# Scores of the first two head pairs: two matmuls a tile on keys where they land, in place of one on laid-out keys

## What is computed

```python
k_sum = k.reshape(B, H, nb, 32, D).max(axis=3)       # maxima of 24 blocks of 32 keys
v_sum = v.reshape(B, H, nb, 32, D).mean(axis=3)
scores_l = scale * q @ k.T        # kept only where |i - j| < 16
scores_s = scale * q @ k_sum.T + log(32)
a = softmax(concat([where(mask, scores_l, -1e9), scores_s]))
x = a @ concat([v, v_sum])
u = x + (x.T @ U @ V).T
x = u + relu(u @ w_ch1) @ w_ch2
xk, xr = mu * x + (1 - mu) * x_prev        # one mu for each
out = sigmoid(xr @ w_r) * (relu(xk @ w_k) ** 2 @ w_v)
```

## Time and profile before

| what | us |
|---|---|
| median of 3 runs | 513.48 (513.07 to 514.33) |
| profiled execution, whole | 515.51 |
| its span, first to last instruction | 513.7 |
| TensorE busy in it | 504.6 (98%) |
| VectorE, ScalarE, GpSimd busy | 255.4, 202.2, 44.7 |

### The profile page before, as it was taken

One profiled execution on the slowest core, in us unless ns is written; L12 is line 12 of the kernel. 1 busy time (PEld: TensorE's weight loads), 2 busy tenths in 40 slices (PEclk: granted clock), 3 DMA queues, 4 the chain that ended last, 5 costly groups with the idle time before them and its releaser, 6 DMA issues.

```text
span 513.7 us, 8595 instructions
## 1 busy us (share of the span) xinstructions
PE 504.6 (98%) x3444; PEld 469.7 (91%) x3444; DVE 255.4 (50%) x594; ACT 202.2 (39%) x403; POOL 44.7 (9%) x63
## 2 busy tenths in 40 slices
PE   7899999999999999999999999999999999999997
PEld 5679899999999999999999999999889889988987
DVE  4666654555445245354453553785544652562501
ACT  5466442432334154141331422554633542561510
POOL 5585320201000000000000000000000000000000
PEclk9699999999999999999999999999999999999999
DMA  8997534112022021133142341400010001001001
GB/s 266 318 280 230 158 105 160 38 47 83 1 83 83 1 84 41 42 124 122 42 132 73 104 142 41 126 1 0 1 41 22 1 22 41 1 1 61 0 1 61
DMA packets 13160, 40.83 MB, mean 79 GB/s; under 512 B 1729, under 2 KB 2241, under 8 KB 13121
## 3 DMA queue, kind: packets, MB, share of 16 engines
q1 hardware_dynamic: 12688, 39.76, 24.5%
q10 hardware_dynamic: 432, 0.52, 0.3%
HBM read 37.13 MB, written 3.15 MB: 78 GB/s over the span
## 4 chain that ended last, share of the span: by engine, by line
PE 92%; DMA 2%; DVE 2%; issue 1%; ACT 1%; SPq 0%; ACTq 0%; DVEq 0%
PE ps L773 89%; DMA vT<-in_vT 2%; PE ps L833 2%; PE ps L776 1%; DVE u_lo L732 1%; ACT xa L529 1%; DVE xa L726 1%; ACT P L428 0%; DVE P L588 0%; ACT m_hi L509 0%; ACT PT L435 0%; SPq L204 0%; DVE mixr L611 0%; DVE mixr L609 0%; DVE yT L694 0%
## 5 line engine op out<-in xcount | busy, mean ns | idle before, releaser
L773 PE MATMUL ps<-u_hi,w_hi 128*128 128x384 f32 x256 | 87.4, 341 | 0.0
L773 PE MATMUL ps<-h_hi,w_hi 128*128 128x384 f32 x256 | 87.1, 340 | 0.0
L773 PE MATMUL ps<-h_hi,w_lo 128*128 128x384 f32 x256 | 85.9, 335 | 0.0
L773 PE MATMUL ps<-h_lo,w_hi 128*128 128x384 f32 x256 | 85.9, 335 | 0.0
L773 PE MATMUL ps<-u_hi,w_lo 128*128 128x384 f32 x256 | 85.9, 335 | 0.0
L773 PE MATMUL ps<-u_lo,w_hi 128*128 128x384 f32 x256 | 85.8, 335 | 0.0
L492 ACT ACTIVATE h_hi<-ps 128x384 fp32r<-128x384 f32 x64 | 31.4, 491 | 118.2 <-PE ps L773 118.1
L689 DVE SCALAR_TENSOR_TENSOR h_lo<-ps,h_hi 128x384 fp32r<-128x384 f32 x64 | 35.7, 557 | 68.6 <-ACT h_hi L492 68.5
L694 DVE TENSOR_TENSOR yT<-ps,yT 128x384 f32<-128x384 f32 x64 | 35.6, 556 | 54.3 <-PE ps L773 54.3
L773 PEld LDWEIGHTS ps<-u_hi,w_hi 128*128 128x128 f32 x256 | 48.0, 188 | 1.8 <-issue 1.5
L773 PEld LDWEIGHTS ps<-h_hi,w_hi 128*128 128x128 f32 x256 | 48.0, 188 | 1.5 <-issue 1.5
(11 more groups left out here) (93 smaller groups left out, 754.8 us busy)
## 6 DMA issues: line engine op xcount, KB each, us to landing
wraw<-in_w SPq DMA_DIRECT2D x42, 512.0 KB, 3.5
vwin<-in_vw SPq DMA_DIRECT2D x8, 580.5 KB, 12.0
kT<-in_kT SPq DMA_DIRECT2D x8, 400.0 KB, 8.2
vT<-in_vT SPq DMA_DIRECT2D x8, 384.0 KB, 11.9
out<-scratch SPq DMA_DIRECT2D x11, 256.0 KB, 2.0
qt<-in_qT SPq DMA_DIRECT2D x6, 384.0 KB, 12.1
U<-in_U SPq DMA_DIRECT2D x1, 384.0 KB, 12.9
V<-in_V SPq DMA_DIRECT2D x1, 384.0 KB, 12.6
```

Source lines behind the costliest of these rows:

```text
L773: return nc.tensor.matmul(o, lhsT, rhs, start=start, stop=stop)
```

## The change

For pairs 0 and 1 (`DIRECT = 2`) a tile's scores are made of two matmuls for each window and head: one of 96 columns that reads the keys in `kT`, and one of 24 columns that reads `kmax`. All 8 of the first kind come first, then all 8 of the second; before the first of those of pair 0 and of pair 1 stands a wait for `kmax_done`. The tile waits for `k_in` in place of the copies. The four copies of ScalarE for pair 0 and the two of GpSimd for pair 1 are gone. Buffers that were free once copied are now free once scored: the load of `kT` of pair 3 waits for scores(2), that of pair 4 for scores(5); block_max(2) and block_max(3) wait likewise. Pairs 2 to 7 do as before, with counts shifted by two.

```diff
+DIRECT = 2
...
             def load_k(p):
                 need(sp, kmax_done, p - NBUF + 1)
-                need(sp, kw_done, p - NBUF)
-                if p == NBUF:
-                    sp.wait_ge(kw0_done, 2)
+                if p >= NBUF:
+                    if p - NBUF < DIRECT:
+                        sp.wait_ge(s_done, UNITS * (p - NBUF + 1))
+                    else:
+                        sp.wait_ge(kw_done, p - NBUF - DIRECT + 1)
                 sp.dma_start(kT[p % NBUF][:, :], kT_in[p]).then_inc(k_in[p % NBUF], 16)
...
             def windows(p):
                 pool.wait_ge(k_in[p % NBUF], 16 * (p // NBUF + 1))
-                need(pool, s_done, UNITS * (p - 1))
+                if p - 2 >= DIRECT:
+                    pool.wait_ge(s_done, UNITS * (p - 1))
...
-            windows(1)
-            spread(0, kw_done, 1, 0, 4)
-            summaries(1)
+            spread(0, zero_ok, 2, 0, 4)
...
-            act.wait_ge(k_in[0], 16)
-            first_windows(0, 8)
-            act.wait_ge(kmax_done, 1)
-            first_summaries(0, 8)
-            first_windows(8, NW)
-            first_summaries(8, NW)
             exps(0)
...
             def block_max(p):
                 dve.wait_ge(k_in[p % NBUF], 16 * (p // NBUF + 1))
-                need(dve, ksum_done, p - 2)
-                if p == 2:
-                    dve.wait_ge(ksum0_done, 2)
+                if p >= 2:
+                    if p - 2 < DIRECT:
+                        dve.wait_ge(s_done, UNITS * (p - 1))
+                    else:
+                        dve.wait_ge(ksum_done, p - 2 - DIRECT + 1)
...
                 if v == 0:
                     pe.wait_ge(q0_in, 16)
-                    pe.wait_ge(kw0_done, 1)
-                    pe.wait_ge(ksum0_done, 1)
+                    pe.wait_ge(k_in[0], 16)
...
-                    pe.wait_ge(kw_done, p)
-                    pe.wait_ge(ksum_done, p)
+                    if p < DIRECT:
+                        pe.wait_ge(k_in[p % NBUF], 16)
+                    else:
+                        pe.wait_ge(kw_done, p - DIRECT + 1)
+                        pe.wait_ge(ksum_done, p - DIRECT + 1)
...
-                for i in range(2):
-                    for j in range(2):
-                        w = 2 * (2 * u + i) + j
-                        for h in range(2):
-                            r = slice(64 * h, 64 * h + 64)
-                            o = ps[HALF * j:HALF * j + HALF, 512 * s_bank(v, h) + COLS * i:512 * s_bank(v, h) + COLS * i + COLS]
-                            last = mm(o, q[r, HALF * w:HALF * w + HALF], k[r, w, :], True, True)
+                pieces = ((0, BAND), (BAND, COLS)) if p < DIRECT else ((0, COLS),)
+                for lo, hi in pieces:
+                    if lo == BAND and u == 0:
+                        pe.wait_ge(kmax_done, p + 1)
+                    for i in range(2):
+                        for j in range(2):
+                            w = 2 * (2 * u + i) + j
+                            for h in range(2):
+                                r = slice(64 * h, 64 * h + 64)
+                                o = 512 * s_bank(v, h) + COLS * i
+                                keys = (k[r, w, :] if p >= DIRECT else kmax[p % 2][r, :] if lo == BAND
+                                        else kT[p % NBUF][r, HALF * w:HALF * w + BAND])
+                                last = mm(ps[HALF * j:HALF * j + HALF, o + lo:o + hi], q[r, HALF * w:HALF * w + HALF], keys, True, True)
                 last.then_inc(s_done, 1)
```

More of the change, by code:

```diff
@@ L142, in build @@
         q0_in, q1_in, small_in, mu_ok, warm_ok = sem("q0_in"), sem("q1_in"), sem("small_in"), sem("mu_ok"), sem("warm_ok")
-        kmax_done, ksum0_done, ksum_done, vm_done = sem("kmax_done"), sem("ksum0_done"), sem("ksum_done"), sem("vm_done")
+        kmax_done, ksum_done, vm_done = sem("kmax_done"), sem("ksum_done"), sem("vm_done")
         vt_in, vsum_done = [sem("vt_in0"), sem("vt_in1")], sem("vsum_done")
-        kw0_done, kw_done, vs_step, vs_ok, mhi_done = sem("kw0_done"), sem("kw_done"), sem("vs_step"), sem("vs_ok"), sem("mhi_done")
+        kw_done, vs_step, vs_ok, mhi_done = sem("kw_done"), sem("vs_step"), sem("vs_ok"), sem("mhi_done")
         s_done, m_done, e_done, t_done, pt_done, pv_done = (sem("s_done"), sem("m_done"), sem("e_done"), sem("t_done"),
@@ L790, in scores @@
                     pe.wait_ge(q0_in, 16)
-                    pe.wait_ge(kw0_done, 1)
-                    pe.wait_ge(ksum0_done, 1)
+                    pe.wait_ge(k_in[0], 16)
                 if v == 1:
                     pe.wait_ge(q_in[0], 16)
-                if v == 2:
-                    pe.wait_ge(kw0_done, 2)
-                    pe.wait_ge(ksum0_done, 2)
                 if v == 3:
```

## The result

The changed kernel takes 515.74 us (median of 11 runs, 514.02 to 517.59), the kernel before 512.98 us (median of 11, 512.20 to 514.80). The ratio is 1.0055, 95% interval 1.0039 to 1.0071: slower by 2.8 us. A second series gave 1.0047 (1.0027 to 1.0068). I had forecast 514.0, with a range to 515.3 and 0.78 on "no change that can be told".

A forecast was written before the change was run, and what follows sets the result against it. The prediction took TensorE's own work as the bound (busy 504.6 of 513.7 us); its only nonzero term, +0.5 us for added passes, on the median 513.48 gave 514.0 us, range 512.6 to 515.3.

The forecast's parts named there:

- The copies: Opening: dropping ScalarE's four and GpSimd's two copies gains 0, as VectorE waits for `vT` anyway; scores(3) starts near 10.8.
- the moved loads: Loads of `kT` of pairs 3 and 4, now waiting for scores(2) and scores(5), were to cost 0.
- my +0.5 us: Forecast cost of the added passes in scores(4) and scores(5) at half clock; bounds 0 and 2.0 us.
- scores(4) and scores(5): Two tiles behind 16.87 us, 32 passes instead of 16: the one term with a price, +0.5 us.
- whatever is added to TensorE behind 16.87 is paid: From times_v(1) at 16.87 us the chain is TensorE almost without a break, so added work there costs time.
- I let it stay at half from 16.87 to 22.4: Opening: TensorE's clock was expected at 0.50 while scores(4) and scores(5) run, returning to 1.00 at 22.4 us.
- rival B: Opening: TensorE's clock doesn't fall at all, 1.8 us won, 511.7 us; chance 0.08.
- those 2.0 us: The profiled execution, 515.51 us, stood 2.0 us above the median of 513.48; the forecast kept that difference, 516.0 against 514.0.
- A to D: Rivals A (opening sets the end, 512.9, chance 0.08), rival B, C, and D (added passes free, 513.5, chance 0.15).
- C: Opening: the clock comes back later than 22.4 us, so 2.0 us slower, 515.5 us; chance 0.13.

The follow-up runs named there:

- experiment 2: The changed kernel with one 120-column matmul per window and head for pairs 0 and 1, straight from landed keys, block maxima left out: 513.20 us, 1.0004 to the kernel before.
- Experiments 3 and 8: The kernel before with small warming matmuls, making 192 and 96 more TensorE instructions respectively: 516.16 us, 1.0058, and 514.63 us, 1.0029.
- experiments 9 to 11: Side by side: changed kernel again, 1.0047 to the kernel before; two matmuls a tile with copies kept, reading the laid-out copy, 1.0027, or landed keys, 1.0026.

## Why the prediction was wrong

**What held.** The copies are worth nothing: `vT` is still what VectorE waits for at 12.39, and experiment 2 gives 1.0004. scores(3) starts at 10.88 (I said 10.8). No run shows a cost of the moved loads. The rule of the Trainium skill ("TensorE: Matmul & The Clock Gate", Part 1) on the spacing of short matmuls gave 0.4 us a tile, as an estimate; the trace has 0.69 - 0.57 = 0.12 for 16 passes, and all 32 passes of scores(3) in 0.69 us are 22 ns apart on average, below that rule's 25. In array time my +0.5 us was too much: two tiles at 0.12 make 0.24, and in the profile after they aren't on the chain.

**The step that failed** is the sum under "scores(4) and scores(5)": "This is the one term with a price." It counts a matmul by the time that it takes in the array. The added ones also take room in TensorE's program, and I put that at nothing without naming it. The opening was close to running short of program already: the stop of 0.32 us at 24.35, inside a tile without a semaphore, stood in the trace of before, and I passed over it. Experiments 3 and 8 take up more room in the program and add no pass behind the warming, and give +0.58% and +0.29%; the whole change is +0.55%. Experiment 2 takes the room back (and the added passes with it), and the loss is gone. In the profiles the waits stand on the chain with 2.06 us (changed kernel) and 2.14 us (the same again), and the added passes of scores(4) and scores(5) with nothing.

**A second step that failed:** "whatever is added to TensorE behind 16.87 is paid". That was read from one execution, in which the `vT` of pair 1 landed at 14.39 and the clock was at half. In the profile after it had landed by 12.39, times_v(1) started at 14.85 (my text has the forecast wrong from before 16 on), and the next `vT`, that of pair 2, became the start of the chain. TensorE waits for it up to 24.04.

**The clock.** I let it stay at half from 16.87 to 22.4. In the profile after, it was full until 34.2 and fell there, behind a wait of 2.06 us. That is rival B in its condition, and yet the kernel was slower, not 1.8 us faster: TensorE was 3.0 us ahead at the transposes of unit 5 and 0.7 us behind at the dense part. Of these 3.7 us 2.06 are the second stop, and the other 1.6 go with the half clock between 34.3 and 37.7. The clock alone isn't the loss: in the series of experiments 9 to 11, runs with a mean clock of 0.999 or more have a median of 514.6 us for the changed kernel (4 runs) and 512.8 for the one before (13 runs).

**The base.** I took the half clock of the profiled execution for the kernel's habit, although the page stood 2.0 us above the median; I carried those 2.0 us along as a constant. The clocks of the runs explain a part of it: the 4 of 35 with a mean clock of 0.993 or less have a median of 514.9 us, the 17 of 0.999 or more one of 512.6. But the latter spread from 511.8 to 514.1 by themselves, so the clock isn't all of it. A profile above the highest of its plain runs should have been a warning.

**The chances.** A loss of 2.8 us was slower than A to D; C had its size (515.5) for another reason. The range ended at 515.3 since it left out most of C, and no cost beside array time and the clock was in it.

## What to carry to other kernels

Cutting matmuls in two costs program as well as array time: in a stretch in which loads fill the transfer engines, look in the trace for an engine that stops inside a batch of equal instructions with no semaphore as its releaser, and count how many instructions it has between such stops. Where one stands there already, an edit that adds instructions ahead of it can cost more than they take in the array. Before a step is called on the path, ask which transfer the chain starts with, and whether the next one would take its place if the first landed sooner. When an interval from one batch to the next is taken as a batch's cost, look at what the second one waited for. And compare the profiled execution with the spread of the plain runs before its clock is taken as given.

## What the runs showed of the hardware

- TensorE's program comes in pieces of 16 KB, one for about 253 loads and matmuls; 19 stops in 10 profiles ended 1.3 to 1.6 us behind the end of such a transfer. They took 0.3 to 2.1 us and all lay ahead of 44 us. In the dense part, with the transfer engines at 0.26 and 12 to 28 us to a piece, there was none.
- 192 added instructions at the start, whose own work was over by 7.3 us, came with 3.1 us of stops at 25 and 34 us.
- Splitting 120 columns into 96 and 24 on 64 x 64 quarters of the array added 0.12 us to a tile of 0.57 us at full clock, 7.5 ns for each of 16 added passes; the 32 passes were 22 ns apart on average.
- One and the same kernel had a mean clock of 0.999 or more in 17 of 35 runs, of 0.996 or 0.997 in 14, and of 0.990 or 0.993 in 4; the first had a median of 512.6 us, the last of 514.9. The profile at 0.990 had 10 us at half clock.
